# Attention with top-32 selection before two MLPs: the first unit's weights and values in full precision, lanes selected one by one, an opening order of its own

## What is computed

```python
scores = scale * np.matmul(q, k.transpose(0, 1, 3, 2))
kth = np.partition(scores, -32, axis=-1)[..., -32:-31]
scores = np.where(scores >= kth, scores, -1000000000.0)
attn = np.exp(scores - np.max(scores, axis=-1, keepdims=True))
attn = attn / (np.sum(attn, axis=-1, keepdims=True) + 1e-09)
x = np.matmul(attn, v)            # then (2304 tokens, 512)
h = x @ w_in                      # 2048 wide
x = (h * sigmoid(h)) @ w_out      # 512
out = ((x @ w1) * (x @ w2)) @ w3 @ w_out2   # 1024 wide, then 512
```

## Time and profile before

| | us |
|---|---|
| median of 3 runs | 1138.74 (1138.3 to 1140.32) |
| the profiled execution | 1139.89 |
| its span, first to last instruction | 1138.0 |
| PE busy in the span | 1056.2 |
| DVE busy | 930.9 |
| ACT busy | 773.0 |
| POOL busy | 621.1 |
| first H on PE (line 995) | starts at 153.5 |
| mean granted clock of PE | 0.984 of full speed |

### The profile page before, as it was taken

The page is one execution under the profiler, slowest core; times in us unless marked ns, Lnnn a source line. Parts: engine busy times, 40 slices in busy tenths (PEclk is TensorE's granted clock), DMA queues, the critical chain, the costliest instruction groups (busy, mean ns, idle before and its releaser), DMA issues.

```text
span 1138.0 us, 24334 instructions
## 1 busy us (share of the span) xinstructions
PE 1056.2 (93%) x7872; PEld 986.5 (87%) x7872; DVE 930.9 (82%) x2066; ACT 773.0 (68%) x1921; POOL 621.1 (55%) x803
## 2 busy tenths in 40 slices
PE   1998577899999999999999999999999999999898
PEld 1554477799999999999999999999999999999897
DVE  5698886798889999999999998989999999991110
ACT  4577767677777787777767777877677767764221
POOL 3566767766665455566645555666545545543211
PEclk9999679999999999999999999999999999999999
DMA  8987769986998599779966996899579847963972
GB/s 270 316 281 250 260 221 311 310 275 200 330 374 288 163 342 346 260 233 359 359 236 212 335 345 212 265 365 362 193 249 335 297 154 279 331 216 128 312 244 93
DMA packets 129053, 310.42 MB, mean 273 GB/s; under 512 B 14240, under 2 KB 43936, under 8 KB 128928
## 3 DMA queue, kind: packets, MB, share of 16 engines
q1 hardware_dynamic: 110112, 275.30, 71.8%
q10 hardware_dynamic: 18816, 33.56, 8.4%
HBM read 263.19 MB, written 45.61 MB: 271 GB/s over the span
## 4 chain that ended last, share of the span: by engine, by line
PE 72%; DMA 9%; POOL 4%; DVE 4%; issue 4%; ACT 4%; ACTq 2%; SPq 1%; POOLq 0%; DVEq 0%
PE ps_h L1033 6%; PE ps_h L1035 6%; PE ps_h L1034 6%; DMA win<-win_split 6%; PE ps_s L929 5%; PE ps_x L965 5%; PE ps_h L995 5%; PE ps_h L996 5%; PE ps_h L997 5%; PE ps_y L1017 4%; PE ps_y L1019 4%; PE ps_y L1018 4%; PE ps_t L944 4%; PE ps_y L1046 3%; PE ps_y L1047 3%
## 5 line engine op out<-in xcount | busy, mean ns | idle before, releaser
L828 DVE MAX8 top<-rest 128x8 f32<-128x576 f32 x432 | 309.9, 747 | 0.0
L639 POOL TENSOR_TENSOR g_lo<-gate,g_hi 128x256 fp32r<-128x256 f32 x216 | 160.0, 741 | 240.7 <-ACT g_hi L796 240.2
L830 DVE MATCH_REPLACE8 rest<-top,rest 128x576 f32<-128x576 f32 x288 | 212.9, 743 | 0.5
L995 PE MATMUL ps_h<-x_hi,win 128*128 128x256 f32 x576 | 167.9, 291 | 9.1 <-DMA win<-win_split 8.9
L1033 PE MATMUL ps_h<-x_hi,w_hi 128*128 128x256 f32 x576 | 166.1, 288 | 5.1 <-DVE x_lo L884 4.4
L627 POOL TENSOR_TENSOR pT<-p_raw,pT 128x640 fp32r<-128x640 f32 x72 | 113.4, 1575 | 103.1 <-ACT pT L756 103.1
L1017 PE MATMUL ps_y<-g_hi,wout 128*128 128x256 f32 x576 | 165.7, 288 | 1.1 <-POOL g_lo L639 1.0
L996 PE MATMUL ps_h<-x_lo,win 128*128 128x256 f32 x576 | 163.0, 283 | 0.0
L997 PE MATMUL ps_h<-x_hi,win 128*128 128x256 f32 x576 | 162.9, 283 | 0.0
L1035 PE MATMUL ps_h<-x_hi,w_lo 128*128 128x256 f32 x576 | 162.7, 282 | 0.0
L1034 PE MATMUL ps_h<-x_lo,w_hi 128*128 128x256 f32 x576 | 162.7, 282 | 0.0
(11 more groups left out here) (78 smaller groups left out, 2840.2 us busy)
## 6 DMA issues: line engine op xcount, KB each, us to landing
win<-win_split SPq DMA_DIRECT2D x135, 512.0 KB, 6.4
wout<-wout_split SPq DMA_DIRECT2D x135, 512.0 KB, 4.9
wout<-w_dram SPq DMA_DIRECT2D x72, 512.0 KB, 3.9
v_split<-v_dram SPq DMA_DIRECT2D x64, 320.0 KB, 5.2
k_split<-k_dram SPq DMA_DIRECT2D x64, 288.0 KB, 5.8
v_dram<-v_split SPq DMA_DIRECT2D x32, 320.0 KB, 6.1
k_raw<-kT SPq DMA_DIRECT2D x64, 144.0 KB, 5.4
k_dram<-k_split SPq DMA_DIRECT2D x32, 288.0 KB, 6.9
```

The lines of the kernel that those rows point to most:

```text
L639: nc.gpsimd.tensor_tensor(g_lo[:, n % NR, :], gate[:, n % NG, :], g_hi[:, n % NR, :].bitcast(F32), ALU.subtract).then_inc(g_split, 1)
L828: nc.vector.max(best[:, 8 * n:8 * n + 8], sc if step == 0 else left).then_inc(topk_step, 1)
L830: nc.vector.match_replace(left, best[:, 8 * n:8 * n + 8], sc if step == 1 else left, BELOW_ALL).then_inc(topk_step, 1)
L995: nc.tensor.matmul(ps_h[:, f % 2, 0:UN], hi, xh, start=(c == 0), stop=False)
```

## The change

- In the first eight steps (unit 0, `FULL_STEPS = 8`) the transposed weights are copied once, as full 32-bit numbers, into `p_full` (in pT's place), and PV takes them and the raw v with five full-precision matmuls. No VR, no LO, no copies into p_raw, no XS for these steps; XC writes the result. Keys are still split.
- Keys and values used in unit 0 are not stored. `comes_raw` loads them raw again in unit 1, where they are split and stored. SP's load of a raw v waits for `pv_ready` in unit 0.
- TOP, and all that follows it, goes lane by lane: the seven steps of a lane stand one after the other, SHIFT on DVE takes the place of POOL's BOUNDS, DEN and RDEN come per lane, and MASK and EXP use another sign and scale (`STEEP = 2.0 ** 90`) with the 32nd value itself as the bias.
- The order of the opening (some two units' worth) is given by explicit places (`FIRST_PLACES`, `in_order`); behind it the order is again by time, with other values of LAG, `M0 = 9.742` and `TOP_SPAN = 1.066` (before 0.754).
- wo2 comes in four parts and W34 waits for each; the second pair of raw MLP weights is loaded later (WSL); Q(1) and V(0) come later on SP; H(u,0) waits for x chunk by chunk.

```diff
-STEEP = 1.0e30
+STEEP = 2.0 ** 90
...
+FULL_STEPS = 8
+ENTRIES = [(s, n, b, s % H) for s in range(STEPS) for n, (b, _, _) in enumerate(segments(s // H))]
...
+def kept(e):
+    return FIRST_USE.get(ENTRIES[e][2:]) == e
+def comes_raw(e):
+    return ENTRIES[e][0] < H or kept(e)
+def v_is_split(e):
+    return comes_raw(e) and not in_full(e)
...
-M0 = 9.887
+M0 = 9.742
...
-TOP_SPAN = 0.754
+TOP_SPAN = 1.066
...
+FIRST_PLACES = {
...
+    "vector": {
+        "SHIFT": (9, 24, 37, 38, 52, 56, 74, 80, 87, 100, 115, 127, 134, 147, 151, 162, 169, 189, 194,
...
+        "G": (214, 220, 221, 226, 234, 254, 259, 263, 270, 278, 285, 293, 302, 311, 314, 320,),
...
+def in_order(engine, out):
+    first, rest, seen = [], [], {}
+    for at, op in sorted(out, key=lambda o: o[1][1:]):
+        places = FIRST_PLACES.get(engine, {}).get(op[0], ())
+        n = seen[op[0]] = seen.get(op[0], -1) + 1
+        if n < len(places) and places[n] >= 0:
+            first.append((places[n], op))
+        else:
+            rest.append((at, op))
+    return sorted(first, key=lambda o: o[0]) + sorted(rest, key=lambda o: o[0])
+def lag(kind, s):
+    return s + (START_LAG if s < H else LAG)[kind]
...
-        for step in range(7):
-            for lane in range(2):
-                out.append((s + TOP_SPAN * (2 * step + lane) / 14, ("TOP", s, step, lane)))
-        out += [(s + LAG[kind], (kind, s)) for kind in ("DEN", "RDEN", "XS")]
-        out += [(s + LAG["LOD"], ("LO", t)) for t in (2 * s, 2 * s + 1) if on_vector(t)]
+        for lane in range(2):
+            out += [(lag("TOP", s) + TOP_SPAN * (7 * lane + step) / 14, ("TOP", 2 * s + lane, step)) for step in range(7)]
+            out.append((lag("TOP", s) + TOP_SPAN * (7 * lane + 6.5) / 14, ("SHIFT", 2 * s + lane)))
+            out += [(lag(f"{kind}{lane}", s), (kind, 2 * s + lane)) for kind in ("DEN", "RDEN")]
+        if s >= FULL_STEPS:
+            out += [(lag("XS", s), ("XS", s)), (lag("LOD", s), ("LO", 2 * s))]
...
+                    if FULL_STEPS + 2 > n >= 2:
+                        sp.wait_ge(pv_ready, n - 1)
+                    elif n >= 2:
+                        sp.wait_ge(v_ready, n - 1 - FULL_STEPS)
...
-                elif kind == "BOUNDS":
...
                 elif kind == "MASK":
...
-                    act.wait_ge(bias_ready, s + 1)
+                    act.wait_ge(topk_step, 7 * t + 7)
...
-                                         bias=bounds[:, s % 2, lane, 1:2], scale=SCALE, alpha=STEEP).then_inc(masked, 1)
+                                         bias=top[:, t % 4, TOPK - 1:TOPK], scale=-1.0, alpha=1.0 / STEEP).then_inc(masked, 1)
...
+                    nc.scalar.activation(probs[:, t % 4, :], probs[:, t % 4, :], ACT.Exp, bias=shift[:, t % 4, :],
+                                         scale=-SCALE * STEEP, accum_out=den[:, t % 4, :]).then_inc(probs_ready, 1)
...
+                    if s < FULL_STEPS:
+                        nc.scalar.copy(p_full[0:D, 2 * KCH - 1, cols], tail(t))
+                        nc.scalar.copy(p_full[:, 0:KCH - 1, cols], ps_t[:, :, :]).then_inc(p_rounded, 1)
+                        continue
...
+                elif kind == "SHIFT":
+                    t = op[1]
+                    dve.wait_ge(topk_step, 7 * t + 7)
...
+                    nc.vector.tensor_scalar(shift[:, t % 4, :], top[:, t % 4, TOPK - 1:TOPK], top[:, t % 4, 0:1], SCALE,
+                                            ALU.subtract, ALU.mult).then_inc(shift_ready, 1)
...
+                    if s < FULL_STEPS:
+                        pe.wait_ge(p_rounded, 2 * s + 2)
+                        pe.wait_ge(v_loaded[s % 2], 16 * (s // 2 + 1))
+                        for c in range(KCH):
+                            rows, at = (P, c) if c < KCH - 1 else (D, 2 * KCH - 1)
+                            m = nc.tensor.matmul(ps_x[0:D, 0:UN], v_raw[0:rows, s % 2, c, :], p_full[0:rows, at, :],
+                                                 start=(c == 0), stop=(c == KCH - 1))
```

More of the change, by code:

```diff
@@ L213, in split_steps @@
     for s in range(STEPS):
[L214 to L217, removed]
+        out.append((lag(q, s), ("QR", s)))
+    for e, (s, _, _, _) in enumerate(ENTRIES):
+        if comes_raw(e):
+            out.append((lag(k, s), ("KR", e)))
+        if v_is_split(e):
+            out.append((lag(v, s), ("VR", e)))
     return out
@@ L227, in act_order @@
         for lane in range(2):
-            out += [(s + LAG[f"{kind}{lane}"], (kind, 2 * s + lane)) for kind in ("SC", "MASK", "EXP", "EV")]
-        out.append((s + LAG["XC"], ("XC", s)))
+            out += [(lag(f"{kind}{lane}", s), (kind, 2 * s + lane)) for kind in ("SC", "MASK", "EXP", "EV")]
+        out.append((lag("XC", s), ("XC", s)))
         if s % 2:
-            out.append((s + LAG["XH"], ("XH", s // 2)))
+            out.append((lag("XH", s), ("XH", s // 2)))
     for m in range(FC2):
@@ L251, in pool_order @@
         for lane in range(2):
-            out += [(s + LAG[f"{kind}{lane}"], (kind, 2 * s + lane)) for kind in ("NORM", "LO")]
-        out.append((s + LAG["BOUNDS"], ("BOUNDS", s)))
+            out += [(lag(f"{kind}{lane}", s), (kind, 2 * s + lane)) for kind in ("NORM", "LO")[:1 if s < FULL_STEPS else 2]]
         if s % 2:
-            out.append((s + LAG["XL"], ("XL", s // 2)))
+            out.append((lag("XL", s), ("XL", s // 2)))
     for (kind, u, f), p in MLP_AT.items():
@@ L260, in pool_order @@
             out.append((p + LAG["GLB"], ("GL", FC12 * u + FC1 + f)))
[L261 removed]
+    return in_order("gpsimd", out)
 def dve_order():
@@ L286, in sp_order @@
     for s in range(2, STEPS):
-        out.append((s + LAG["Q"], ("Q", s)))
-    for e, (s, _, _, _, fresh) in enumerate(ENTRIES):
+        out.append((lag("Q", s), ("Q", s)))
+    for e, (s, _, _, _) in enumerate(ENTRIES):
         if e < 1:
             continue
[L291 to L296, removed]
+        raw = comes_raw(e)
+        out += [(lag("K" if raw else "KB", s), ("K", e)), (lag("V" if raw else "VB", s), ("V", e))]
+    for e, (s, _, _, _) in enumerate(ENTRIES):
+        if kept(e):
+            out += [(lag("KS", s), ("KS", e)), (lag("VS", s), ("VS", e))]
+    for n in range(W34_PARTS):
+        out.append((-5 + 0.1 * n, ("WO2", n)))
     for m in range(FC2):
-        out.append((-0.6 + 0.25 * m, ("W3", m)))
+        out.append((-5.01 if m == 0 else -0.6 + 0.25 * m, ("W3", m)))
+    out += [(-4.9, ("Q", 1)), (-4.8, ("V", 0))]
     for (kind, u, f), p in MLP_AT.items():
@@ L816, in _ @@
                 if kind == "TOP":
[L817 to L819 removed]
+                    t, step = op[1:]
+                    sc, left, best = scores[:, t % 4, :], rest[:, t % 2, :], top[:, t % 4, :]
                     if step == 0:
                         dve.wait_ge(scores_copied, t + 1)
[L822 to L823 removed]
+                        if t >= 4:
+                            dve.wait_ge(masked, t - 3)
+                            dve.wait_ge(shift_ready, t - 3)
                     else:
[L825 removed]
+                        dve.wait_ge(topk_step, 7 * t + step)
                     n = step // 2
@@ L969, in _ @@
                     m_, part = op[1], op[2]
-                    if m_ == 0 and part == 0:
-                        pe.wait_ge(wo2_loaded, 32)
+                    if m_ == 0:
+                        pe.wait_ge(wo2_loaded[part], 16)
                     if part == 0:
```

239 lines of the change are left out of this document (133 added, 106 removed), and 82 rows, old and new, of tables (FIRST_PLACES, LAG, START_LAG).

## The result

The changed kernel takes 1152.56 us (median of 4 runs, 1148.76 to 1156.46) where the kernel before takes 1139.53 (4 runs, 1138.3 to 1141.98): ratio 1.0112, 95% interval 1.0073 to 1.015. It is slower, by 1.1%. The profiled execution took 1148.76 (span 1147.0), so 9.0 us of span more than before. The forecast was 1126 with a range of 1106 to 1152: wrong in sign, and the median lies just outside.

A forecast was written before the change was run, and what follows sets the result against it. The prediction took DVE to bound the opening and PE the steady part, DVE close behind. Opening -15, second stretch -9.5 and one-batch units +12 gave -12.5 on 1139.9, so 1127.4, with a median of 1126 us; range 1106 to 1152.

The forecast's parts named there:

- the second stretch: From G(0,0) to G(1,0): predicted 116 us, the middle of 106 and 125.5, a gain of 9.5.
- two signs of being wrong: The prediction is wrong if G(0,0) stays after 150 us, or if every later interval passes 115.
- The lower bound: From G(0,0) to G(1,0): 106 us, DVE's 103.3 of work and 2.8 of waits.
- The upper bound: From G(0,0) to G(1,0): 125.5 us as now, if the gate's wait stays with ACT and POOL.
- The opening: Up to G(0,0): 142 us instead of 156.9, taken as -15, mainly from LO, its wait and XS dropped.
- rival 2: Opening's removed wait returns for scores or W34's sums, costing the 15 us again: 1141 us; chance 0.08.
- One-batch stretches: Beside one-batch units DVE becomes the bound: 110.9 us each, +12 over three intervals.
- The rule of the Trainium skill: DVE's search: successive instructions drain the pipe anyway, a semaphore adds nothing; 7.2 us a unit would be nothing.
- Two-batch stretches: Beside two-batch units PE stays the bound: DVE's 108.1 + 2.8 stays under 114 us, so 0.
- Rival 1: DVE bounds every unit; two-batch units lose +14 over three, total 1150 to 1170 us; chance 0.26.
- The new PV: Full-precision PV in the opening: two records a matmul, 2.3 us a step against 1.2, hidden beside DVE.
- Last stretch: The stretch into unit 8: 81 search steps, not 112, so 0 change.

The follow-up runs named there:

- the serial search alone: The kernel before with one edit, the seven search steps of a lane one after the other, all other order unchanged: 1155.28 us, ratio 1.012.
- the old order: The changed kernel's computation in the order of the kernel before (alternating lanes, old times, no explicit places): 1150.34 us, ratio 1.0076.
- staggered: The changed kernel with two lanes searched alternately from lane 38 on, nothing left out: 1136.91 us, ratio 0.995 against the kernel before.

## Why the prediction was wrong

**The step that failed** is the second stretch, "I take the middle, 116". It was 131.5, which is 15.5 of the 21.5 us between the predicted span (1138.0 - 12.5 = 1125.5) and the measured 1147.0. (The medians lie 5 us further apart, because the profiled execution lay 1.2 above its median before and 3.8 below it now.) Neither of the two signs of being wrong that the prediction names would have caught it: the first gate came before 150, and not every later interval passed 115. Two things were wrong in it.

- The lower bound. "106 (work and 2.8 of waits)" is DVE's work alone. PE is busy 111.3 us in that stretch before, and the least of all runs was 110.4 (the serial search alone, at 0.99 of the clock). 116 would have asked PE to lose 9 of its 13.7 us of idle time, and I had named nothing that takes it away: over all runs it was 11.9 to 16.2.
- The upper bound. I took "as now" for it and so excluded a loss, though the change moves sixteen splittings into this stretch. I booked these at nothing "beside a POOL that is idle 45%". That share is of the whole span. In this stretch POOL's work rose from 86.1 to 95.7 us, and POOL's k_split, pT and wout stand one behind the other on the chain to PE's stop at 177 us. In the old order the keys' move costs 4.5 us; in the changed order keeping them gains 2.7 to 2.9. That POOL's place in the chain is the reason is not shown: cutting its key subtractions alone gave 1.2 us, no more than scatter, and which part of the move costs the time (POOL, ACT's casts, the loads and stores) stays open.

The 6.0 us over the kernel before are 4.8 of busy time at the lower clock and 1.2 of idle time. What set them off is known only in sum: 6.6 to 8.0 us come back when POOL and the hand-over of w1 and w2 are lightened together. That the keys are a part of it rests on four comparisons of single executions, which all point the same way (2.7 to 5.8 us, the largest with the values kept too). How the rest divides between the hand-over and POOL is not settled, since each share is as small as the scatter. Why some 12 us of idle time stay in every version was not found.

**The other 6 us**, term by term:

- *The opening* was predicted at 142 and came at 145.7. Waits were 12.7 + 5 = 17.7, measured 18.3. The rest, 3 us, is work: SHIFT took 0.13 instead of 0.07, 1.2 us for 20 of them; the other 2 were not found. But the reason was incomplete. In the old order most of the removed LO and its wait is given back as waits for scores and W34's sums, and 6.0 us from the first search step on are left; the changed kernel has 9.7 there, with the explicit order and the serial search besides, and 1.4 from its earlier start. I had given this 0.08 as rival 2, which shows in the old order and not in the changed kernel.
- *One-batch stretches*: +12 predicted, +11.7 measured, DVE idle 0 to 1.0 us in them. The price of 0.11 us for a waiting neighbour was right: 0.66 to 0.68 became 0.78 to 0.80. The other 2.8 us of waits I had added to DVE's 108.1 did not come; DVE's real work was 110.4, with SHIFT at 0.13 (1 us a unit) and small slots as the likely rest. Right sum, one term too large and one too small. The stretch into unit 5 has another cause besides.
- *The rule of the Trainium skill*, page VectorE: DVE Perf Modes, section The DRAIN you can't avoid, was read in the prediction as having the serial search for nothing, because a semaphore adds nothing there. The trace disagrees with that sentence for the search: 0.77 to 0.80 us to a neighbour that waits, 0.66 to 0.68 to one that doesn't. It agrees with another one of the same section, which the prediction left out, that an instruction which isn't held starts earlier, as the independent neighbours do here. The runs with the dependences away or covered are 1.9 and 1.6% faster than the changed kernel by their ratios to the kernel before (0.9921 and 0.995 against 1.0112).
- *Two-batch stretches*: 0 predicted, -0.2, +1.6, -0.3. Rival 1 needed +14 there and did not come; it had the sign and the size of the result in good part for a wrong reason. Only its second stretch, no shorter than before, came true.
- *The new PV* shows two records a matmul, as expected, ten of them in 2.5 us a step against the 2.3 of the sum.
- *Last stretch*: 0 predicted, +2.4. I argued from 81 search steps instead of 112, but 46 uncovered dependences (5 us) still stand there; staggered it takes 100.5.

## What to carry to other kernels

Bound a stretch by the busy time of every engine in that stretch, and ask which removed wait would take idle time from the one that leads; a middle between two bounds is no forecast, and where work moves into a stretch its upper bound is above today. A search like this one, a chain of dependent instructions on DVE, wants a stranger between two links, but only where the inputs are early enough: serial in the opening and staggered in the steady part gave the version that beat both kernels. Removed work on one engine shows up as time only as far as the next input is early as well: here 6 of 23 us in the old order. And a run that is to isolate one part of a change has to be read from its start, since a load that it issues earlier can hide the gain.

## What the runs showed of the hardware

- A waiting neighbour on DVE starts 0.02 to 0.04 us behind the end of the instruction ahead, an independent one 0.08 before it (after a MAX8 of 0.76 us 0.78 to 0.80 against 0.67); 65 of these in a unit moved the bound from PE to DVE.
- Stops of PE cost more than their idle time, through the clock: in three kernels with 845 to 846 matmuls in the second stretch PE was busy 116.1, 111.3 and 110.9 us at a granted clock of 0.93, 0.98 and 0.99, while its idle time was 14.9, 13.7 and 12.1. In the first of them the clock was at 0.50 to 0.69 in the stretches around stops of 3.1, 3.8 and 2.2 us.
